# An attention and MLP kernel on one core: zero products ahead of and between TensorE's first work, the tail keys' transfers on semaphores of their own, keys swapped ahead of values in four rounds

## The reference, cut to what matters

```python
q_rot, k_rot = rotate(q), rotate(k)                      # [4, 8, 576, 64]
scores = matmul(q_rot, k_rot.transpose(0, 1, 3, 2)) / sqrt(64)
attn = exp(scores - max(scores)); attn = attn / (sum(attn) + 1e-9)
x = matmul(attn, v)                                      # then back to [4, 576, 512]
x = x + relu(layernorm(x) @ w_ch1) @ w_ch2               # first MLP
out = x + gated_mlp(x)                                   # second MLP, with a spatial product over positions
```

## Time and profile before

| What | Value |
|---|---|
| Time, median of 3 runs | 931.07 us (930.28 to 931.92) |
| Time of the profiled execution | 931.98 us |
| Its span, first to last instruction | 930.2 us |
| TensorE busy | 905.6 us, 97% |
| VectorE, ScalarE, GpSimd busy | 705.7, 543.7, 551.0 us |
| Granted TensorE clock, mean | 0.999 |

### The profile page before, as it was taken

One profiled execution on the slowest core, in us unless ns is written; L12 is line 12 of the kernel. 1 busy time (PEld: TensorE's weight loads), 2 busy tenths in 40 slices (PEclk: granted clock), 3 DMA queues, 4 the chain that ended last, 5 costly groups with the idle time before them and its releaser, 6 DMA issues.

```text
span 930.2 us, 18233 instructions
## 1 busy us (share of the span) xinstructions
PE 905.6 (97%) x6153; PEld 840.1 (90%) x6153; DVE 705.7 (76%) x1155; ACT 543.7 (58%) x1184; POOL 551.0 (59%) x547
## 2 busy tenths in 40 slices
PE   4999999999999999999999999999999999999998
PEld 3899999999989999999899988899988989989897
DVE  4799899999998899942777878789998672663623
ACT  3899999999889666543655655565565221212110
POOL 4989899999883477665566668758986210010100
PEclk9999999999999999999999999999999999999999
DMA  6233333334314233100000000002200001010011
GB/s 181 68 98 94 83 93 96 82 93 97 84 43 113 70 96 120 35 1 1 1 1 1 1 1 1 1 2 68 90 26 1 1 1 46 1 50 8 1 47 57
DMA packets 49737, 45.51 MB, mean 49 GB/s; under 512 B 18880, under 2 KB 39616, under 8 KB 49536
## 3 DMA queue, kind: packets, MB, share of 16 engines
q1 hardware_dynamic: 49232, 44.26, 17.4%
q10 hardware_dynamic: 432, 0.30, 0.1%
HBM read 28.81 MB, written 4.72 MB: 36 GB/s over the span
## 4 chain that ended last, share of the span: by engine, by line
PE 85%; DVE 9%; ACT 2%; issue 2%; DMA 1%; SPq 1%; ACTq 0%; DVEq 0%
PE fc_ps L2145 16%; PE seven_ps L2175 14%; PE ring_ps L2041 8%; PE wide_ps L2344 6%; PE scores_ps L1977 6%; PE bank_ps L2300 5%; PE wide_ps L2323 5%; PE bank_ps L2358 5%; PE ring_ps L1988 5%; PE seven_ps L2225 2%; DVE lefts L1651 2%; PE seven_ps L2145 2%; DVE hid_sums L1639 2%; PE scores_ps L1970 2%; PE ring_ps L1923 2%
## 5 line engine op out<-in xcount | busy, mean ns | idle before, releaser
L2145 PE MATMUL fc_ps<-xT,W1s 128*128 128x512 f32 (+1 forms) x828 | 191.0, 380 | 0.4 <-ACT hid L1159 0.3
L2175 PE MATMUL seven_ps<-rights,lefts 128*128 128x256 f32 x1344 | 173.6, 284 | 0.0
L2175 PEld LDWEIGHTS seven_ps<-rights,lefts 128*128 128x128 f32 x1344 | 169.5, 191 | 4.4
L2145 PEld LDWEIGHTS fc_ps<-xT,W1s 128*128 128x128 f32 x828 | 146.2, 189 | 27.7 <-ACT hid L1159 1.3
L1465 DVE TENSOR_REDUCE nmax<-scores_ps 128x1 f32<-128x576 f32 x144 | 106.4, 749 | 17.8 <-PE scores_ps L1977 11.7
L958 POOL TENSOR_TENSOR rights<-w_rest,rights 128x256 fp32r<-128x256 f32 x84 | 80.9, 963 | 54.6 <-ACT rights L1202 54.6
L1065 ACT ACTIVATE E<-scores_ps,nmax 128x576 f32<-128x576 f32 x128 | 95.4, 747 | 10.7 <-DVE nmax L1465 9.9
L1474 DVE TENSOR_TENSOR prob_lo<-ring_ps,prob_hi 128x512 fp32r<-128x512 f32 x144 | 95.3, 681 | 2.4 <-ACT prob_hi L1079 1.9
L1020 POOL TENSOR_TENSOR rstd<-ve,power 128x1 f32<-128x1 f32 x18 | 14.5, 807 | 138.7 <-DVE ve L1833 138.7
L1977 PE MATMUL scores_ps<-stack 128*128 128x288 f32 x384 | 90.0, 321 | 1.2 <-DMA swapped_k<-stack 0.8
L1079 ACT ACTIVATE prob_hi<-ring_ps 128x512 fp32r<-128x512 f32 x144 | 85.3, 610 | 6.4 <-PE ring_ps L1988 5.7
(11 more groups left out here) (185 smaller groups left out, 2066.0 us busy)
## 6 DMA issues: line engine op xcount, KB each, us to landing
swapped_k<-stack SPq DMA_DIRECT2D x32, 144.0 KB, 2.5
stack<-stack SPq DMA_DIRECT2D x32, 144.0 KB, 2.4
w_raw<-in_w SPq DMA_DIRECT2D x18, 256.0 KB, 3.0
qk_raw<-in_k SPq DMA_DIRECT2D x16, 256.0 KB, 2.8
v_raw<-in_v SPq DMA_DIRECT2D x16, 256.0 KB, 2.8
qk_raw<-in_q SPq DMA_DIRECT2D x15, 256.0 KB, 2.8
w_rest<-in_w SPq DMA_DIRECT2D x7, 512.0 KB, 4.5
out<-out_sb SPq DMA_DIRECT2D x14, 256.0 KB, 2.3
```

Of the source, the lines that this page charges most:

```text
L2145: mm = nc.tensor.matmul(fc1_bank(n, f)[:, 0:cols], W1s[:, slot1(f), w, c, :], xT[:, x, c, 0:cols], start=first, stop=(c == DC - 1 and x == 1))
L2175: mm = nc.tensor.matmul(seven_ps[k][:, 2 * P * a:2 * P * (a + 1)], lefts[:, k, x, P * a:P * (a + 1)], rights[:, k, w, :], start=(g == 0 an ...
```

## The change

There are three edits.

1. TensorE issues products of a 128x128 and a 128x512 block of zeros into `ring_ps` bank 0, which nothing else uses in that round: 24 before its first transpose, 2 at the end of round -1 (behind K0 of pair 0), and in round 0 3 behind TL, 4 behind Q0, 4 behind Q1, 2 behind each of the score tiles 1, 2 and 3 ahead of the next, and 1 behind each of two transpose groups. The zeros are a part of `stack` that pair 1 writes later; VectorE clears it with a memset of 128x512 as its first instruction.
2. The three transfers of tail keys count on a semaphore `tails_swapped` of their own. Score tile 4 waits for the swapped keys before its first product, and for the tails only before its second half.
3. Where the round is below 4, SyncE swaps the keys of head 1 before it loads the values.

```diff
+        tails_swapped = [sem(f"tails_swapped{odd}") for odd in range(2)]
+        zeros = stack[:, 1, QMAIN[0]:QMAIN[0] + MAIN]
...
-                    sp.dma_start(stack[:, p.odd, KEYS[1] + S:KEYS[1] + S + TAIL].bitcast(f32), tail).then_inc(keys_swapped[h][p.odd], 16)
+                    sp.dma_start(stack[:, p.odd, KEYS[1] + S:KEYS[1] + S + TAIL].bitcast(f32), tail).then_inc(tails_swapped[p.odd], 16)
                     for half in range(2):
                         to, src = D * half, D * (1 - half)
-                        sp.dma_start(swapped(p, h, S, TAIL)[to:to + D].bitcast(f32), tail[src:src + D]).then_inc(keys_swapped[h][p.odd], 16)
+                        sp.dma_start(swapped(p, h, S, TAIL)[to:to + D].bitcast(f32), tail[src:src + D]).then_inc(tails_swapped[p.odd], 16)
...
             def body(r):
                 load_qk(r + 2, 1)
-                load_values(r)
-                swap_keys(r, 1)
+                if r.ends[1] < LOOP[0]:
+                    swap_keys(r, 1)
+                    load_values(r)
+                else:
+                    load_values(r)
+                    swap_keys(r, 1)
...
+            nc.vector.memset(zeros.bitcast(f32), 0.0).then_inc(zeroed_stack, 1)
...
-                    count = 16 if h == 0 else 40
-                    pe.wait_ge(keys_swapped[h][p.odd], p.i * count + (2 * count - count * p.odd))
+                    pe.wait_ge(keys_swapped[h][p.odd], p.i * 16 + (32 - 16 * p.odd))
...
                     for half in range(2):
+                        if half == 1:
+                            pe.wait_ge(tails_swapped[p.odd], p.i * 24 + (48 - 24 * p.odd))
...
+            def idle(count):
+                for _ in range(count):
+                    nc.tensor.matmul(ring_ps[0][:, :], zeros[:, 0:P], zeros, start=True, stop=True)
+            pe.wait_ge(zeroed_stack, 1)
+            idle(24)
             pe.wait_ge(ident_ready, 1)
             def body(r):
                 make_stack_tails(r)
+                if is_round(r, 0):
+                    idle(3)
...
                 make_stack(r, 0, 0)
+                if is_round(r, 0):
+                    idle(4)
                 score(r - 1, 8)
                 make_stack(r, 1, 0)
+                if is_round(r, 0):
+                    idle(4)
...
                 score(r, 6)
                 make_stack(r + 1, 0, 1)
+                if is_round(r, -1):
+                    idle(2)
```

More of the change, by code:

```diff
@@ L278, in attention_and_mlps @@
         zeroed_rows = sem("zeroed_rows")
+        zeroed_stack = sem("zeroed_stack")
         qk_in = [[sem(f"q_in{odd}"), sem(f"k_in{odd}")] for odd in range(2)]
@@ L2111, in body @@
                 transpose_group(r, 0, 2)
+                if is_round(r, 0):
+                    idle(1)
                 times_v(r - 1, 0, 0, range(2, NTT))
```

## The result

The changed kernel is slower: 933.95 us (median of 20 runs, 931.9 to 935.82) against 931.5 us (20 runs), a ratio of 1.0026 with a 95% interval of 1.0020 to 1.0032. That is 2.5 us lost where 2.4 were forecast as gained. The profiled execution took 932.94 us, with a span of 931.1, so it shows less of the loss than the median does. It is still plain where the loss is.

| | TL of pair 1 | 2 | 3 | 4 | 5 | 6 |
|---|---|---|---|---|---|---|
| before | 28.49 | 46.64 | 63.96 | 81.29 | 99.38 | 116.92 |
| after | 26.91 | 45.20 | 62.94 | 82.16 | 99.84 | 117.45 |
| after minus before | -1.58 | -1.44 | -1.02 | +0.87 | +0.46 | +0.53 |

A forecast was written before the change was run, and what follows sets the result against it. TensorE, busy 97% of the span, was taken as the bound. 1.51 + 1.32 + 0.43 - 0.90 = 2.36 us gained gave 929.6 profiled, 928.7 us median; own range 928.0 to 929.5, overall range 927.2 to 931.3.

The forecast's parts named there:

- The 24 products ahead of all: Before TensorE's first transpose: zero products raise the clock some 5.7 us in and end at about 9.6 us, costing nothing.
- Rival 5: At the start: products of zeros do not raise the clock, so the kernel is slower, 935.4 us; chance 0.07.
- The pace of round 0, and GpSimd as the next limit: Round 0 runs at 2.4 GHz; then GpSimd's split, ending at 26.93, sets TL of pair 1 at 26.98.
- The term of 1.51 us: TL of pair 1 moves from 28.49 to 26.98: 1.51 us gained, bounds 0 and 1.51.
- Swap before values, round 1: Score tile 4 of pair 1 no longer waits for swapped tails: 1.32 us gained, bounds 0 and 1.32.
- Separate semaphores: Score tile 4 of round 4 no longer waits for the last tail transfer: 0.43 us gained, bounds 0 and 0.43.
- The values come late: Rounds 1 to 3: ScalarE's split waits for values, part is taken up: 0.9 us lost, bounds 0 and 2.1.
- Rival 2: Rounds 1 to 3: the values' delay is passed on wholly, 2.1 us lost, giving 929.9 us; chance 0.15.
- Rival 4: Clock falls again in TensorE's gaps between 23.9 and 27.0, round 1 starts at 1.2 GHz: 931.1 us; chance 0.08.

The follow-up runs named there:

- c: The kernel before with the zero products alone (edit 1): 931.95 us, 1.0003 of before.
- b: The changed kernel without edit 3, so zero products and own semaphores with the values loaded first: 930.16 us, 0.9982 of before.
- e: The changed kernel with keys swapped ahead of values in round 1 only; rounds 2 and 3 load values first: 930.56 us, 0.9993 of before.
- k: The changed kernel with keys ahead of values in round 1 only and VectorE's addition of 1e-9 left out: 930.23 us, 0.9979 of before.
- h2: Second measurement of the changed kernel without edit 3 and without VectorE's addition of 1e-9: 928.39 us, 0.9966 of before.
- d: The kernel before with the separate semaphores for tail keys alone (edit 2): 930.08 us, 0.9983 of before.
- j: The whole changed kernel with VectorE's addition of 1e-9 left out: 932.37 us, 1.0013 of before.
- a: The kernel before with edit 3 alone, keys swapped ahead of values where the round is below 4: 934.41 us, 1.0032 of before.
- f: The changed kernel with ScalarE's split of values moved behind score tile 4's exponential and the read-out, in all rounds: 935.77 us, 1.0050 of before.
- h: The changed kernel without edit 3 and without VectorE's addition of 1e-9, first measurement: 927.77 us, 0.9966 of before.

## Why the prediction was wrong, by its own steps

- **The 24 products ahead of all.** Right: forecast to end at 9.6, ended at 9.9, and the clock rose under them (24 in 8.63 us). Rival 5 is out.
- **The pace of round 0, and GpSimd as the next limit.** Right in the profile: TL of pair 1 at 26.91 where 26.98 was forecast, with a wait for GpSimd. The term of 1.51 us was mis-sized at its other end. I took 28.49 of one trace for what the kernel does without the products; its clock had risen late, and other traces have 27.2 to 28.95. The zero products alone measured 1.0003 of before: nothing.
- **Swap before values, round 1: 1.32 us.** This step failed. The wait at score tile 4 did go, but the time was not freed. The prediction asked of GpSimd only when its split of pair 2 was ready (42.55 against 43.8), and not which operation of VectorE waits for its end. VectorE's addition could not run until 42.55, and the read-out of TensorE's bank stands behind it. The gap at score tile 4 had covered that. And the gap itself came from one slow issue, 2.78 us for the two loads of values, which the prediction took for the rule; with the zero products it is 1.12 and there is no gap to close (c). Kernels b and e, without and with this step, take 930.16 and 930.56, and without the addition it costs 1.8 us (k against h2).
- **Separate semaphores: 0.43 us.** Right in kind, too small: 1.5 us. In the profile of d, round 4 is 0.73 us shorter than before and round 1 0.92; the latter may be a faster issue of the values (1.64 us and not 2.78) as well as the semaphores, these runs don't part them. And the tail transfers are late now and then in other rounds, as in the profile of c, where TensorE lost 1.0 us at score tile 4 in round 3.
- **The values come late: 0.9 us.** This is the largest error: 3.4 us in rounds 2 and 3 alone. The lateness was forecast at 0.6, 0.6 and 0.9 us, against 0.80, 0.39 and 1.89: near enough in rounds 1 and 2, half of it in round 3, and up to 1.86 and 1.98 in round 2 of j and round 1 of k. What failed besides is the statement that a part is taken up. I followed the delay to K0, behind VectorE's `prob_lo`. Ahead of that, the transpose of the query tails needs the bank that `o_pair` frees, and it has no slack: 1.89 us of wait on ScalarE became 1.43 on TensorE and 1.89 us of a longer round. Rival 2 (passed on wholly) had the mechanism, with too small a stall. In round 3, a pause of 0.4 us in SyncE's issue and a slow landing came on top, which the round before had not shown.
- **Rival 4** did happen, in b and c, between 27.9 and 31.1 us, but cost nothing there: round 1 was tied to GpSimd's end in any case. Among the executions of the changed kernel those with the lower mean clock are 1.4 us longer, which may be this rival. The Trainium skill, "TensorE: Matmul & The Clock Gate", section "Why this matters for your kernels", warned of just this idleness, and the granted clock of 0.50 in b agrees.

In sum, from medians taken in different series: forecast -1.51 - 1.32 - 0.43 + 0.90 = -2.4; measured about 0 for the zero products, -1.5 for the semaphores, +3.8 for the order (933.95 - 930.16), together +2.3.

## What to carry to other kernels

A load that is moved behind other transfers must be followed to every engine that has it in a fixed order, and from there to the first bank it keeps, not to the one that looks likely: in a pipeline whose bottleneck has no slack, a stall of the second engine is passed on whole. When a wait is removed, look at what ran on time only because of it; here a 0.15 us operation on VectorE turned into 2.9 us beside GpSimd. And a wait or a start that was seen in one trace should be read from several before a gain is put on it: here the clock rose at another time in each trace, and the gap of 1.32 us hung on one slow DMA issue.

## What the hardware showed that I had not expected

- A VectorE addition of 128x9 between two SBUF tensors takes 0.15 us, and up to 2.9 us when GpSimd works, mostly 1.0 to 1.1; wherever it was long, in all rounds of before, after and a to f, it ended 0.01 to 0.04 us behind a GpSimd operation's end. A reciprocal of the same size is not held: in h it took 0.20 us at 39.87, while GpSimd worked without a pause from 38.51 to 42.73. Leaving the addition out gave 1.5 to 2.4 us of 930.
- The clock was at 2.4 GHz from 17.8 to 21 us in one execution without zero products, fell, and rose again by 24.6; in others it rose once, between 23 and 27 us. The same program thus comes to TL of pair 1 at 27.22 or at 28.95, though of these 1.7 us up to 1.0 is GpSimd's later start.
